# 64x64 score products, and queries and keys loaded with six tokens to a partition, in an attention and mixing kernel

## The chip, the cores and the metric

The kernel runs on one core of a Trainium2 chip. The time is that of the device in microseconds, the median of several runs of the whole kernel.

## The reference

Three stages follow each other: a windowed attention with block summaries, a token and channel mixing, and a second channel mixing. The change lies in the first.

```
# q, k, v: (2, 8, 768, 64)
k_sum = k.reshape(B, H, nb, 32, D).max(axis=3)          # nb = 24
v_sum = v.reshape(B, H, nb, 32, D).mean(axis=3)
scores_l = scale * q @ k^T, kept where |i - j| < 16, else -1e9
scores_s = scale * q @ k_sum^T + log(32)
a = softmax(concat[scores_l, scores_s])
out = a @ concat[v, v_sum]
...
h = relu(x^T @ w_tok1) @ w_tok2;  u = x + h^T
u = u + relu(u @ w_ch1) @ w_ch2
...
r = sigmoid(xr @ w_r);  out = r * (relu(xk @ w_k)^2 @ w_v)
```

## The kernel before, in words

The program writes out each engine's instructions in order and joins them by semaphores. Everything is in one core's memory; all DMAs are issued by SP, in one queue.

The attention goes over eight pairs of heads (`p`, with buffers `par` = p % 2). A pair has 12 units of 64 queries; a unit sees 96 keys of its window and 24 summary keys, 120 columns. Four units make a group `r` (three to a pair, `G` counts them through). For a pair the steps are:

- SP loads keys and queries, `load_qk` (L301), each head by itself into `kn` and `qn`: a partition gets two neighbouring tokens in each of three blocks of 256. It also loads the values, `load_v8` (L315, 96 rows of 512 floats) for the summaries and `load_vw` (L310, rows of 64 floats, windows of the values), and spreads the summed values over the units from chip memory, `spread_vs` (L321). L351 loads a piece of the weights of the mixing.
- TensorE transposes three blocks a head (`turn_k`, `turn_q`, L895) into `bK` and `bQ`. The rows of the result are token parity times the 64 features, so the copies out of PSUM take 64 rows at a time.
- DVE (L665) and ACT (L506) copy the keys to `kt`, head 0 in rows 0 to 63, head 1 in rows 64 to 127. DVE takes block maxima (`summary_keys`, L669) and cuts the windows (`cut_windows`, `add_summaries`) into `kw`. ACT copies the queries (`turn_out_q`, L498) to `qbd`, a block diagonal of both heads, whose other half stays zero from two memsets at the start (L654).
- TensorE multiplies `qbd` with `kw` (`scores`, L928), 128x128 weights for both heads of a unit, into one of two banks `bS`. DVE adds the mask and takes the negated maximum (`maxima`, L693); ACT takes exponentials (`exps`, L518). TensorE transposes them (L976) into one of two banks `bT`, ACT copies them to `aT` (L551), and TensorE multiplies by the values (L998, called AV below). DVE divides by the row sums.

On TensorE the steps of iteration `p` are, for each `r`: transposes of the exponentials of G, scores of G + 3, `turn_k` of pair p + 2 (r = 0) or `turn_q` (r = 1), the summary of the values (L918, r = 2), then AV of G. In the last two pairs products of the next stage (`hidden_tiles`, L946 to L948) fill in. SP's iteration `p` waits for the value summary of pair p to be copied, then issues L321, the loads L301 of pair p + 2 (4), L315 (2), L310 of pair p + 1 (6) and L351:

```
def pair(p, par, i=None):
    sp.wait_ge(qbank_read, 5 * p + 5)
    spread_vs(par)
    ...
        load_qk(p + 2, par)
        ...
        load_v8(p + 2)
    sp.wait_ge(av_done, 3 * p + 1)
    load_vw(p + 1, 1 - par)
```

TensorE's, SP's, ACT's and DVE's code for pairs 0 to 5 is a loop of three rounds over two pairs; the last two pairs are written out.

Of the kernel before, what the change touches and what calls it, by code (L numbers as in the profile page):

```python
# [18 lines left out]
def build_program(nc, q, k, v, w_tok1, w_tok2, w_ch1, w_ch2, mu_k, mu_r, w_k, w_v, w_r, out):  # L19
    B, NH, S, D = q.shape  # L20
    P = 128
# [31 lines left out]
    with ctx:  # L53
# [62 lines left out]
        qbd = [reg.take(f"qbd{i}", [P, NU, P]) for i in range(2)]  # L116
# [4 lines left out]
        qn = [reg.take(f"qn{i}", [P, 2, NB, P]) for i in range(2)]  # L121
        kn = [reg.take(f"kn{i}", [P, 2, NB, P]) for i in range(2)]
# [53 lines left out]
        bS, bT, bA, bQ, bK = bank[0:2], bank[2:4], bank[4:6], bank[6], bank[7]  # L176
# [120 lines left out]
        def _(sp):  # L297
            def load_qk(p, par):
                for dst, src, loaded in ((kn, k_rows, ld_k), (qn, q_rows, ld_q)):
                    for h in range(2):  # L300
                        sp.dma_start(dst[par][:, h, :, :],  # L301
                                     src[bass.ds(2 * p + h, 1)].rearrange("o p t n -> (o p) t n")
                                     ).then_inc(loaded[par], 16)
# [33 lines left out]
            def pair(p, par, i=None):  # L337
                sp.wait_ge(qbank_read, 5 * p + 5)
# [18 lines left out]
            sp.wait_ge(qbank_read, 5 * NP)  # L357
# [130 lines left out]
        def _(act):  # L488
            def turn_out_q(pp, par, h, free, banks=(bQ, bK)):


                act.wait_ge(q_turned, 2 * pp + h + 1)
                if free is not None and h == 0:
                    act.wait_ge(scores_done, free)
                for j in range(2):
                    dst = qbd[par][h * D:h * D + D, :, h * D + j:h * D + D:2]
                    src = banks[h][j * D:j * D + D, 0:NB * P].rearrange("p (u i) -> p u i", i=UQ // 2)
                    act.activation(dst, src, ACT.Copy, scale=float(D) ** -0.5).then_inc(qbank_read, 1)  # L498

            def turn_out_k(pp, free):  # L500
# [4 lines left out]
                for j in range(2):  # L505
                    act.activation(kt[D:2 * D, WIN + j:WIN + S:2], bQ[j * D:j * D + D, 0:NB * P],  # L506
                                   ACT.Copy).then_inc(kt_written, 1)
# [20 lines left out]
            act.activation(warm[:, :], qbd[0][0:D, 0, D:D + 1], ACT.Exp)  # L528
            turn_out_k(0, None)
            for h in range(2):  # L530
                turn_out_q(0, 0, h, None, bT)
# [12 lines left out]
            def pair(p, par, prep):  # L544
                for r in range(NG):
# [5 lines left out]
                    act.activation(aT[gp][:, :, :].rearrange("p u n -> p (u n)"), bT[gp][0:COLS, :],  # L551
# [72 lines left out]
            act.wait_ge(init_dve, 6)  # L624
# [27 lines left out]
        def _(dve):  # L652
            for par in range(2):
                dve.memset(qbd[par][:, :, :], 0.0).then_inc(init_dve, 1)  # L654
# [5 lines left out]
            def turn_out_k(pp, j, free):  # L660
# [4 lines left out]
                dve.tensor_copy(kt[0:D, WIN + j:WIN + S:2], bK[j * D:j * D + D, 0:NB * P]).then_inc(kt_written, 1)  # L665

            def summary_keys(pp):
                dve.wait_ge(kt_written, 4 * pp + 4)
# [14 lines left out]
            def maxima(G, r, par, free):  # L683
# [51 lines left out]
            for j in range(2):  # L735
                turn_out_k(0, j, None)
# [3 lines left out]
            maxima(0, 0, 0, None)  # L740
            maxima(1, 1, 1, None)
            for j in range(2):
                turn_out_k(1, j, 2)
# [3 lines left out]
            maxima(2, 2, 0, None)  # L747
# [9 lines left out]
            for part in range(2):  # L757
# [3 lines left out]
                for par in range(2):  # L761
                    p = 2 * i + par
                    for r in range(NG):
                        G, gp = 3 * p + r, (3 * par + r) % 2
                        if part == 0 or par == 0:
                            maxima(G + 3, r, 1 - gp, GU * G + GU)
# [6 lines left out]
                        if part == 0 and r == 0:  # L773
                            turn_out_k(p + 2, 0, 2 * p + 4)
# [370 lines left out]
```

## Time and profile before

| | |
|---|---|
| median of 3 runs | 504.31 us (503.15 to 505.6) |
| profiled execution, its span | 501.4 us |
| TensorE busy | 478.4 us (95%) |
| DVE busy | 221.7 us (44%) |
| ACT busy | 191.6 us (38%) |
| DMA | 48657 packets, 31.70 MB |

The profiled execution has no time of its own besides its span, from the first to the last instruction; the median of the runs is 2.9 us above it. The busy shares are means over stages that differ much: the attention takes the first fifth of the span. How a stage is bound is read from the windows of that stage, the queue of SP over time, and the chain of waits that ended last.

### The profile page before, as it was taken

What the parts mean: (1) busy time and instruction counts of PE and PEld (TensorE: products, weight loads), DVE (VectorE), ACT (ScalarE), POOL (GpSimd) and SP (SyncE); (2) the same over time, 40 slices, a digit from 0 to 9 for tenths busy, and PEclk for the clock granted to TensorE, in tenths of its full rate; (3) what the DMA queues carried; (4) which work ended last, traced back from release to release, by engine and by line L of the source; (5) the groups of instructions that cost most, each with busy time, mean ns of one, the idle gap of its engine ahead of it and who ended that gap; (6) DMA issues with size and microseconds to landing.
All of it is one profiled execution on the core that took longest, in us unless ns stands there. A gap on an engine that the chain in (4) does not pass through costs nothing.

```text
span 501.4 us, 8399 instructions
## 1 busy us (share of the span) xinstructions
PE 478.4 (95%) x2968; PEld 444.9 (89%) x2968; DVE 221.7 (44%) x575; ACT 191.6 (38%) x424; POOL 114.6 (23%) x98
## 2 busy tenths in 40 slices
PE   4798789998999999999999999999999999999996
PEld 4677678787999999999999999999889989989985
DVE  5598887499411141114111411456436355444521
ACT  3799887424211121112111211345455256353411
POOL 6364553285999000000000024300000000000000
PEclk9999999999999999999999999999999999999999
DMA  9999997144443100000000010000010001001001
GB/s 196 181 208 215 228 213 186 46 126 129 166 149 145 43 1 0 0 0 0 0 0 0 0 42 0 0 1 0 1 49 14 0 21 42 0 0 63 0 0 63
DMA packets 48657, 31.70 MB, mean 63 GB/s; under 512 B 21248, under 2 KB 42496, under 8 KB 48640
## 3 DMA queue, kind: packets, MB, share of 16 engines
q1 hardware_dynamic: 48640, 31.49, 26.4%
q8 instruction: 9, 0.15, 0.1%
q14 instruction: 8, 0.07, 0.1%
HBM read 27.14 MB, written 3.15 MB: 60 GB/s over the span
## 4 chain that ended last, share of the span: by engine, by line
PE 84%; SPq 5%; DMA 5%; ACT 2%; issue 2%; DVE 1%; POOL 0%; ACTq 0%; POOLq 0%
PE bank L946 26%; PE bank L947 26%; PE bank L948 26%; DMA kn<-in_k_dram 4%; SPq L301 2%; PE bank L998 1%; SPq L310 1%; DMA v<-in_v_dram 1%; PE bank L976 1%; ACT e_sb L518 1%; PE bank L1017 1%; ACT qbd L498 1%; PE bank L895 1%; SPq L321 1%; PE bank L928 1%
## 5 line engine op out<-in xcount | busy, mean ns | idle before, releaser
L845 DVE SCALAR_TENSOR_TENSOR rL<-bank,rH 128x384 fp32r<-128x384 f32 x48 | 26.7, 557 | 148.2 <-ACT rH L614 148.2
L614 ACT ACTIVATE rH<-bank 128x384 fp32r<-128x384 f32 x48 | 23.6, 492 | 163.1 <-PE bank L948 158.7
L946 PE MATMUL bank<-uH,W1H 128*128 128x384 f32 x192 | 64.8, 337 | 0.0
L947 PE MATMUL bank<-uL,W1H 128*128 128x384 f32 x192 | 64.6, 336 | 0.0
L948 PE MATMUL bank<-uH,W1L 128*128 128x384 f32 x192 | 64.4, 336 | 0.0
L947 PE MATMUL bank<-xkL,WkH 128*128 128x384 f32 x128 | 43.3, 338 | 0.0
L946 PE MATMUL bank<-xkH,WkH 128*128 128x384 f32 x128 | 43.1, 337 | 0.0
L948 PE MATMUL bank<-xkH,WkL 128*128 128x384 f32 x128 | 42.8, 335 | 0.0
L947 PEld LDWEIGHTS bank<-uL,W1H 128*128 128x128 f32 x192 | 36.1, 188 | 0.0
L948 PEld LDWEIGHTS bank<-uH,W1L 128*128 128x128 f32 x192 | 36.0, 188 | 0.0
L946 PEld LDWEIGHTS bank<-uH,W1H 128*128 128x128 f32 x192 | 36.0, 188 | 0.0
L482 POOL CAST W2aH<-stg 128x1024 fp32r<-128x1024 f32 x3 | 3.1, 1040 | 142.3 <-PE bank L948 142.3
L871 DVE SCALAR_TENSOR_TENSOR k<-bank,kr 128x384 f32<-128x384 f32 x32 | 17.8, 556 | 38.7 <-ACT kr L631 38.6
L948 PE MATMUL bank<-rH,W2aL 128*128 128x384 f32 x96 | 32.3, 336 | 0.0
L948 PE MATMUL bank<-rH,W2bL 128*128 128x384 f32 x96 | 32.3, 336 | 0.0
L946 PE MATMUL bank<-rH,W2bH 128*128 128x384 f32 x96 | 32.2, 335 | 0.0
L947 PE MATMUL bank<-rL,W2bH 128*128 128x384 f32 x96 | 32.2, 335 | 0.0
L946 PE MATMUL bank<-rH,W2aH 128*128 128x384 f32 x96 | 32.2, 335 | 0.0
L947 PE MATMUL bank<-rL,W2aH 128*128 128x384 f32 x96 | 32.2, 335 | 0.0
L631 ACT ACTIVATE kr<-bank 128x384 f32<-128x384 f32 x32 | 15.7, 489 | 43.1 <-PE bank L948 42.7
L518 ACT ACTIVATE e_sb<-s_sb,nmx 128x120 f32<-128x120 f32 x96 | 29.7, 382 | 3.3 <-DVE nmx L693 3.3
L928 PE MATMUL bank<-kw,qbd 128*128 128x120 f32 x192 | 27.6, 292 | 1.8 <-ACT qbd L498 1.6
(131 smaller groups left out, 1093.2 us busy)
## 6 DMA issues: line engine op xcount, KB each, us to landing
stg<-in_moe_w_ch_dram SPq DMA_DIRECT2D x12, 512.0 KB, 3.6
vw<-in_v_dram SPq DMA_DIRECT2D x16, 240.0 KB, 4.9
kn<-in_k_dram SPq DMA_DIRECT2D x16, 192.0 KB, 3.8
qn<-in_q_dram SPq DMA_DIRECT2D x16, 192.0 KB, 4.4
v<-in_v_dram SPq DMA_DIRECT2D x16, 192.0 KB, 5.1
out_dram<-o_sb SPq DMA_DIRECT2D x12, 256.0 KB, 2.0
stg<-in_moe_w_k_dram SPq DMA_DIRECT2D x4, 512.0 KB, 3.5
stg<-in_moe_w_v_dram SPq DMA_DIRECT2D x4, 512.0 KB, 3.4
```

The source lines that it names most:

```text
L301: sp.dma_start(dst[par][:, h, :, :], src[bass.ds(2 * p + h, 1)].rearrange("o p t n -> (o p) t n")).then_inc(loaded[par], 16)
L310: sp.dma_start(dst, src[bass.ds(2 * p + h, 1)].rearrange("o p t n -> (o p) t n")).then_inc(ld_vw[par], 16)
L321: sp.dma_start(vw[par][LOC:COLS, :, :, :].rearrange("p t h n -> p t (h n)"), vsb[par][:, :, :].rearrange("p h n -> p (h n)").unsqueeze(1) ...
L518: act.activation(e_sb[par][:, n, :], s_sb[r][:, n, :], ACT.Exp, bias=nmx[:, r, n:n + 1], scale=-1.0).then_inc(exp_done, 1)
L614: act.activation(rH[f % 2][:, :], bank[f % 2][:, 0:GR], ACT.Relu).then_inc(rh_done, 1)
L631: act.activation(kr[f % 2][:, :], bank[f % 2][:, 0:GR], ACT.Relu).then_inc(kr_done, 1)
L845: dve.scalar_tensor_tensor(out=rL[f % 2][:, :], in0=bank[f % 2][:, 0:GR], scalar=0.0, in1=rH[f % 2][:, :].bitcast(F32), op0=ALU.max, op1=A ...
L871: dve.scalar_tensor_tensor(out=k2[f % 2][:, :], in0=bank[f % 2][:, 0:GR], scalar=0.0, in1=kr[f % 2][:, :], op0=ALU.max, op1=ALU.mult).then ...
L928: ins = pe.matmul(bS[gp][:, COLS * n:COLS * n + COLS], qbd[par][:, t, :], kw[par][:, t, :], start=True, stop=True)
L946: pe.matmul(dst, wH, mH, start=start, stop=False, **more)
L947: pe.matmul(dst, wH, mL, start=False, stop=False, **more)
L948: return pe.matmul(dst, wL, mH, start=False, stop=stop, **more)
```

## The change

The diff has six parts. (1) A partition of `kn` and `qn` now holds six neighbouring tokens with both heads side by side, so a load of one head brings pieces of 64 floats. (2) A transposed block has the features of head 0 in rows 0 to 63 and of head 1 in rows 64 to 127, so one copy brings out 128 rows; the copy puts every sixth token (`in_order`). Keys: one copy by DVE and one by ACT, queries: two by ACT. (3) `qT` holds the plain queries, with no zeros, and the memsets go. (4) A score product becomes two of 64x64 weights, one a head; unit n odd has the heads' output rows swapped, which AV takes into account. (5) The scores have three banks, `bT` one; a group's scores wait for half of the maxima of the group before (`GU * (G + 2) + 2`) in place of all of those of the group before that (`GU * (G + 1) + GU`). (6) TensorE's loop over pairs is written out in full. Semaphore counts follow.

```diff
-        qbd = [reg.take(f"qbd{i}", [P, NU, P]) for i in range(2)]
+        qT = [reg.take(f"qT{i}", [P, S]) for i in range(2)]
...
-        qn = [reg.take(f"qn{i}", [P, 2, NB, P]) for i in range(2)]
-        kn = [reg.take(f"kn{i}", [P, 2, NB, P]) for i in range(2)]
+        qn = [reg.take(f"qn{i}", [P, NB, 2, 2, D]) for i in range(2)]
+        kn = [reg.take(f"kn{i}", [P, NB, 2, 2, D]) for i in range(2)]
...
-        bS, bT, bA, bQ, bK = bank[0:2], bank[2:4], bank[4:6], bank[6], bank[7]
+        bS, bT, bA, bQ, bK = bank[0:3], bank[3], bank[4:6], bank[6], bank[7]
+
+        def score_bank(r, n):
+
+            return bS[(2 * r + n % 2) % 3]
...
-        heads = "b h (t p j) d -> (b h) p t (j d)"
-        q_rows = q.rearrange(heads, t=NB, j=2)
-        k_rows = k.rearrange(heads, t=NB, j=2)
+        heads = "b h (p j) d -> (b h) p (j d)"
+        q_rows = q.rearrange(heads, j=2 * NB)
+        k_rows = k.rearrange(heads, j=2 * NB)
+
+        def turned_block(src, half, blk):
+
+            i = NB * half + blk
+            return src[:, i // 2, i % 2, :, :].rearrange("p h d -> p (h d)")
+
+        def in_order(ap, half):
+
+            return ap.rearrange("q (p i) -> q i p", i=2 * NB)[:, NB * half:NB * half + NB, :]
...
-                        sp.dma_start(dst[par][:, h, :, :],
-                                     src[bass.ds(2 * p + h, 1)].rearrange("o p t n -> (o p) t n")
+                        sp.dma_start(dst[par][:, :, :, h, :].rearrange("p t j d -> p (t j) d"),
+                                     src[bass.ds(2 * p + h, 1)].rearrange("o p (i d) -> (o p) i d", d=D)
...
-                for j in range(2):
-                    dst = qbd[par][h * D:h * D + D, :, h * D + j:h * D + D:2]
-                    src = banks[h][j * D:j * D + D, 0:NB * P].rearrange("p (u i) -> p u i", i=UQ // 2)
-                    act.activation(dst, src, ACT.Copy, scale=float(D) ** -0.5).then_inc(qbank_read, 1)
+                dst = in_order(qT[par][:, :], half)
+                act.activation(dst, columns(banks[half], dst), ACT.Copy, scale=float(D) ** -0.5).then_inc(qbank_read, 1)
...
-            for par in range(2):
-                dve.memset(qbd[par][:, :, :], 0.0).then_inc(init_dve, 1)
...
-                for n in range(GU):
-
-
-                    dve.tensor_tensor_reduce(out=s_sb[r][:, n, :], in0=bS[par][:, COLS * n:COLS * n + COLS],
+                for n in (0, 2, 1, 3):
+                    c = COLS * (n // 2)
+                    dve.tensor_tensor_reduce(out=s_sb[r][:, n, :], in0=score_bank(r, n)[:, c:c + COLS],
...
-                    t = GU * r + n
-                    ins = pe.matmul(bS[gp][:, COLS * n:COLS * n + COLS], qbd[par][:, t, :], kw[par][:, t, :],
-                                    start=True, stop=True)
+                    t, c = GU * r + n, COLS * (n // 2)
+                    for h in range(2):
+                        rows, to = slice(h * D, h * D + D), slice((h + n) % 2 * UQ, (h + n) % 2 * UQ + UQ)
+                        ins = pe.matmul(score_bank(r, n)[to, c:c + COLS], qT[par][rows, t * UQ:t * UQ + UQ],
+                                        kw[par][rows, t, :], start=True, stop=True)
...
-                        scores(p + 1, 1 - par, r, 1 - gp, GU * (G + 1) + GU)
+                        scores(p + 1, 1 - par, r, GU * (G + 2) + 2)
...
-            with pe.Fori(0, NP // 2 - 1) as i:
-                for par in range(2):
-                    pair(2 * i + par, par, True)
-            for par in range(2):
-                pair(NP - 2 + par, par, False)
+            for p in range(NP):
+                pair(p, p % 2, p < NP - 2)
```

What SP issues at the head of its loop over the pairs (`vw_72` and `kn_77` are the buffers of even pairs; ISA and REGISTER_ALU rows are waits and register work). Before:

```order
L321 DMA vw_72<-vsb_83 24x12x130
L341 ISA
L301 ISA
L301 DMA kn_77<-in_k_dram 128x3x128
L301 ISA
L301 DMA kn_77<-in_k_dram 128x3x128
L301 DMA qn_75<-in_q_dram 128x3x128 x2
L344 REGISTER_ALU
L315 DMA v_79<-in_v_dram 96x512 x2
```

and now:

```order
L334 DMA vw_72<-vsb_83 24x12x130
L354 ISA
L314 ISA
L314 DMA kn_77<-in_k_dram 128x6x64
L314 ISA
L314 DMA kn_77<-in_k_dram 128x6x64
L314 DMA qn_75<-in_q_dram 128x6x64 x2
L357 REGISTER_ALU
L328 DMA v_79<-in_v_dram 96x512 x2
```

The order is the same; each load of keys or queries has six pieces of 64 floats a partition in place of three of 128.

On ACT, from the copy of the keys to the copy of the third group's transposed exponentials, in the loop over the pairs. Before:

```order
L506 ACTIVATE kt<-bank 64x384 x2
L551 ACTIVATE aT_88<-bank 120x512
L515 ISA
L518 ACTIVATE e_sb_86<-s_sb_89,nmx 128x120 x4
L492 REGISTER_ALU
L498 ACTIVATE qbd_68<-bank 64x12x32 x4
L551 ACTIVATE aT_87<-bank 120x512
```

and now:

```order
L521 ACTIVATE kt<-bank 128x3x128
L565 ACTIVATE aT_88<-bank 120x512
L529 ISA
L532 ACTIVATE e_sb_86<-s_sb_89,nmx 128x120 x4
L509 REGISTER_ALU
L513 ACTIVATE qT_68<-bank 128x3x128 x2
L565 ACTIVATE aT_87<-bank 120x512
```

Two copies of keys are one, four of queries are two, each with 128 rows; nothing else moves.

On TensorE, the first iteration over a pair, from the first group's transposes. Before, in the loop:

```order
L976 MATMUL bank<-ident,e_sb_85 120x128 x4
L922 ISA
L923 ISA
L925 ISA
L928 MATMUL bank<-kw_71,qbd_69 128x120 x4
L901 ISA
L903 ISA
L895 MATMUL bank<-ident,kn_77 128x128 x6
L991 ISA
L992 ISA
L998 MATMUL bank<-vw_72,aT_87 64x65 x8
L976 MATMUL bank<-ident,e_sb_86 120x128 x4
```

and now, written out:

```order
L988 MATMUL bank<-ident,e_sb_85 120x128 x4
L940 MATMUL bank<-kw_71,qT_69 64x120 x8
L905 MATMUL bank<-ident,kn_77 128x128 x6
L1011 MATMUL bank<-vw_72,aT_87 64x65 x8
L988 MATMUL bank<-ident,e_sb_86 120x128 x4
L940 MATMUL bank<-kw_71,qT_69 64x120 x8
```

Four score products of a group are eight, with 64 rows of output each, in the same places, and the waits and register rows of the loop are gone or carried by the products.

## Rows read from the trace of the kernel before

**Rows 1.** The page: span, slices of TensorE and of DMA, DMA packets.

```profile
span 501.4 us, 8399 instructions
...
PE   4798789998999999999999999999999999999996
...
DMA  9999997144443100000000010000010001001001
...
DMA packets 48657, 31.70 MB, mean 63 GB/s; under 512 B 21248, under 2 KB 42496, under 8 KB 48640
```

**Rows 2.** The timeline of SP, its queue: start us, us, line, transfer, count.

```profile
16.57 1.02 SPq L301 DMA_DIRECT2D kn<-in_k_dram  x2
...
26.21 1.31 SPq L301 DMA_DIRECT2D kn<-in_k_dram  x2
...
56.99 1.13 SPq L301 DMA_DIRECT2D kn<-in_k_dram  x2
...
60.49 3.59 SPq L310 DMA_DIRECT2D vw<-in_v_dram  x6
...
65.97 1.16 SPq L301 DMA_DIRECT2D kn<-in_k_dram  x2
```

**Rows 3.** The views of L301, L310, L321: ns of one issue, min/median/max.

```profile
L301 SPq DMA_DIRECT2D kn<-in_k_dram x16: 387/438/645, 0.8 to 66.6; - x16
...
L310 SPq DMA_DIRECT2D vw<-in_v_dram x48: 317/374/2298, 6.0 to 81.3; - x48
...
L321 SPq DMA_DIRECT2D vw<-vsb x8: 822/840/997, 15.2 to 81.9; - x8
```

**Rows 4.** Waits of SP from 0 to 100 us: in total, times, longest.

```profile
SPq L321 <- ACT qbd L498: 3.3, 4, 0.9
```

**Rows 5.** Waits of TensorE from 20 to 80 us: in total, times, longest.

```profile
PE bank L895 <- DMA kn<-in_k_dram: 4.1, 5, 1.6
```

**Rows 6.** One round, by windows: busy of PE, PEld, DVE, ACT, POOL; clock; DMA.

```profile
46.00:57.00 11.00, 9.24 (x106) 7.94 (x106) 9.04 (x42) 9.40 (x26) 5.79 (x6) 1.00 1.23 211
```

**Rows 7.** The chain that ended last, 60 to 98 us: start, us, what.

```profile
66.62 4.77 DMA kn<-in_k_dram
...
75.41 0.43 ACT qbd L498
...
76.95 0.52 ACT qbd L498
...
79.46 0.89 PE bank L928 x8
```

**Rows 8.** The same chain in the first 32 us.

```profile
5.55 5.95 DMA v<-in_v_dram
```

**Rows 9.** Windows by what is in flight; the last figure is GB/s.

```profile
2.00:6.00 4.00, 1.51 (x6) 1.14 (x6) 2.62 (x7) 1.11 (x3) 3.25 (x12) 1.00 0.88 254
...
10.00:12.00 2.00, 2.00 (x11) 2.00 (x11) 0.33 (x3) 0.00 (x0) 0.43 (x1) 1.00 1.39 177
...
39.00:41.00 2.00, 1.68 (x19) 1.43 (x15) 1.37 (x7) 1.94 (x8) 0.81 (x1) 1.00 1.16 274
...
53.00:55.00 2.00, 1.94 (x22) 1.69 (x18) 1.60 (x5) 1.88 (x6) 0.57 (x1) 1.00 1.34 198
...
81.00:83.00 2.00, 2.00 (x26) 1.52 (x25) 1.80 (x12) 0.62 (x3) 1.33 (x2) 1.00 0.99 206
...
86.00:88.00 2.00, 2.00 (x26) 1.56 (x24) 1.03 (x9) 2.00 (x7) 0.00 (x0) 1.00 0.99 337
```

**Rows 10.** Groups of instructions, 0 to 170 us: count, busy us, mean ns.

```profile
L498 ACT ACTIVATE qbd<-bank 64x384 f32<-64x384 f32 x32 | 16.6, 519 | 1.7 <-PE bank L895 1.2
...
L665 DVE COPY kt<-bank 64x384 f32<-64x384 f32 x16 | 8.9, 555 | 4.3 <-PE bank L895 3.0 <-issue 0.9
...
L588 ACT ACTIVATE u<-bank 128x384 f32<-128x384 f32 x16 | 7.9, 492 | 14.3 <-PE bank L1017 14.3
...
L693 DVE CUSTOM_DVE_ANT_0 s_sb<-bank,mask 128x120 f32<-128x120 f32 x96 | 21.2, 276 | 6.8 <-ACT e_sb L518 3.1 <-PE bank L928 2.8 <-issue 0.8
```

More of the change, by code:

```diff
@@ L488, in _, with columns, turn_out_q @@
         def _(act):
-            def turn_out_q(pp, par, h, free, banks=(bQ, bK)):
-                act.wait_ge(q_turned, 2 * pp + h + 1)
-                if free is not None and h == 0:
+            def columns(bank, dst):
+                src = bank[:, 0:NB * P]
+                return src if len(dst.shape) == 2 else src.rearrange("q (i p) -> q i p", i=NB)
+            def turn_out_q(pp, par, half, free, banks=(bQ, bK)):
+                act.wait_ge(q_turned, 2 * pp + half + 1)
+                if free is not None and half == 0:
                     act.wait_ge(scores_done, free)
-                for j in range(2):
-                    dst = qbd[par][h * D:h * D + D, :, h * D + j:h * D + D:2]
-                    src = banks[h][j * D:j * D + D, 0:NB * P].rearrange("p (u i) -> p u i", i=UQ // 2)
-                    act.activation(dst, src, ACT.Copy, scale=float(D) ** -0.5).then_inc(qbank_read, 1)
+                dst = in_order(qT[par][:, :], half)
+                act.activation(dst, columns(banks[half], dst), ACT.Copy, scale=float(D) ** -0.5).then_inc(qbank_read, 1)
             def turn_out_k(pp, free):
@@ L504, in turn_out_k @@
                     act.wait_ge(kw_ready, free)
-                for j in range(2):
-                    act.activation(kt[D:2 * D, WIN + j:WIN + S:2], bQ[j * D:j * D + D, 0:NB * P],
-                                   ACT.Copy).then_inc(kt_written, 1)
+                dst = in_order(kt[:, WIN:WIN + S], 1)
+                act.activation(dst, columns(bQ, dst), ACT.Copy).then_inc(kt_written, 1)
             def turn_out_vs(p, par):
@@ L526, in _ @@
             act.wait_ge(init_dve, 1)
-            act.activation(warm[:, :], qbd[0][0:D, 0, D:D + 1], ACT.Exp)
+            act.activation(warm[:, :], kt[0:D, 0:1], ACT.Exp)
             turn_out_k(0, None)
             for h in range(2):
-                turn_out_q(0, 0, h, None, bT)
+                turn_out_q(0, 0, h, None, bA)
             exps(0, 0, 0)
@@ L681, in add_summaries, with maxima @@
                                 ks[:, :].unsqueeze(1).to_broadcast([P, NU, NSUM])).then_inc(kw_ready, 1)
-            def maxima(G, r, par, free):
+            def maxima(G, r, free):
                 dve.wait_ge(init_pool, 4)
@@ L733, in high_wt @@
                 dve.tensor_copy(hi, halves(stg[par][:, 0:512])).then_inc(wh_done, 1)
-            for j in range(2):
-                turn_out_k(0, j, None)
+            turn_out_k(0, None)
             summary_keys(0)
@@ L739, in _ @@
             add_summaries(0, 0)
[L740 to L743, printed above, removed]
+            maxima(0, 0, None)
+            maxima(1, 1, None)
+            turn_out_k(1, 2)
             summary_keys(1)
@@ L746, in _ @@
             add_summaries(1, 1)
-            maxima(2, 2, 0, None)
+            maxima(2, 2, None)
             dve.wait_ge(ld_mu, 32)
@@ L765, in _ @@
                         if part == 0 or par == 0:
-                            maxima(G + 3, r, 1 - gp, GU * G + GU)
+                            maxima(G + 3, r, GU * G + GU)
                         if part == 1 and 3 * par + r == 2 * NG - 1:
@@ L779, in _ @@
                         invert(G, r)
-                        if part == 0 and r == 0:
-                            turn_out_k(p + 2, 1, 2 * p + 4)
-                        elif part == 0 and r == 1:
+                        if part == 0 and r == 1:
                             cut_windows(par, 3 * p + 3)
@@ L892, in _, with turn @@
         def _(pe):
-            def turn(src, dst):
+            def turn(src, half, dst):
                 for blk in range(NB):
-                    ins = pe.transpose(dst[:, blk * P:blk * P + P], src[:, blk, :], ident[:, :])
+                    ins = pe.transpose(dst[:, blk * P:blk * P + P], turned_block(src, half, blk), ident[:, :])
                 return ins
```

56 lines of the change are left out of this document (30 added, 26 removed).

## Prediction

> **What bounds the kernel now.** I began with the page [rows 1]. TensorE stands at 9 in nearly every slice of the span, but not in the first eight, and there the DMA row stands at 9 six times and once at 7; after that it falls. The change touches only the attention, which lies in the first eight slices (100 us), so the question is what ends last there.
>
> Next the queue of SP over time [rows 2]. From 16.6 us on it issues without a pause: a round for one pair of heads is four loads of queries and keys (L301), two of L315, six of L310, one of L351, one of L321, and then the next L301. Of five rounds the first begins with L301 at 26.21 and the last at 65.97 us: 39.76 us for four rounds, 9.94 us each. In the shortest, from 56.99, the six L310 take 3.59 us, though a typical one needs 0.374 us [rows 3], 2.2 us for six: SP is held back inside L310, even there. The list of SP's waits [rows 4] has 3.3 us on ACT in four waits and little else, while TensorE in the same stretch waits for `kn` to land [rows 5]. In one round (46 to 57 us) the 16 DMA engines show a share of 1.23 (over 1, since packets overlap) at 211 GB/s, and DVE and ACT are busy 9.0 and 9.4 us of 11 [rows 6]. So the DMA engines set the pace of the attention, ACT stands close behind, and TensorE's products cost nothing there. This holds until the keys of the last pair land at 71.4 us; the chain then runs over ACT and TensorE [rows 7]. The chain of the first 32 us says the same of the start: it is the eight loads L301 and one of L315, then 5.95 us until `v8` lands behind them [rows 8], then POOL, TensorE, ACT and L321.
>
> **The change, part by part.**
>
> *Loads.* Each `kn`/`qn` load still moves 128 x 384 x 4 = 196.6 kB, but as 128x6x64 in place of 128x3x128: 768 pieces of 256 B in place of 384 of 512 B. Over 32 loads that is 12,288 more packets. The trace has both sizes. Where L301's loads are in flight the rate is 254 GB/s at the start and 274 at 39 to 41 us; where it is L310, whose rows are 64 floats (256 B), the rate is 177 GB/s in the first of four windows and 198 in the last, mean of the four 185.5 [rows 9]. A load takes 0.77 and 0.72 us by the first pair, 0.75 on average, and 1.06 by the second: **+0.31 us a load**. The upper end is 1.11 less 0.72, 0.39; the lower is from 81 to 83 us, where 256 B rows arrive with no queue behind them at 206 GB/s: 0.95 less 0.75, 0.20. I take 0.31, since the loads run in a full queue as those windows do.
>
> The Trainium skill ("DMA: Bandwidth & Descriptors", Why small descriptors are slow) counts 11 cycles for a 256-byte descriptor, 3 of them fixed; by the same count 512 bytes take 19, so two small ones cost 22 against 19. That would be an estimate of +0.12 us a load and, with the other terms below, 506.8 us. The rows differ from it by more, 185.5 against some 264 GB/s, and I go by the rows; the page's Specifications ("≥512 B" for line rate) do agree with them.
>
> How many loads count: eight stand ahead of `v8` in the first chain (8 x 0.31 = 2.5 us), and 22 from the restart at 16.57 us to the keys of the last pair (five pairs of four, then two): 6.8 us. Together **+9.3 us**.
>
> *Issue.* The other cost of a load is SP's time. L301 takes 0.438 us; L321, a form whose two sides don't split alike, takes 0.840 [rows 3]. The new loads may stay at the first or go to the second, as their source is now one row of 768 pieces; then +0.40 us each. The shortest round, from 56.99 to 65.97, has 9.0 us, of which 3.59 - 2.24 = 1.35 is the hold in L310 [rows 2, 3]; the other 7.6 and 1.6 more make 9.2 us, under the 9.94 + 4 x 0.31 = 11.2 us that the DMA engines need. So I cost it at nothing, hidden by the drain; at the start 8 x 0.40 = 3.2 would take the place of 2.5.
>
> *Copies out of PSUM.* ACT's four copies of queries become two, its two of keys one; DVE's two become one. Now one of queries takes 519 ns and one of DVE's 555 [rows 10]; ACT's copies of keys have the form of the first. The new ones have 128 rows by 384 and write at a step of six elements. Below: 492 ns, the contiguous 128x384 copy of L588 [rows 10]; above I allow twice 519, since no row has this step. At 519 a round saves 3 x 0.52 on ACT, 0.56 on DVE, all under cover of the loads, which is why I count none of it for the rounds. In the last round the chain holds all four L498, from 75.41 to 77.47 us [rows 7]: two fall away, **-1.0 us**. The keys' copy there isn't in the chain. At twice the price the term is 0.
>
> *Score products.* Per group of four units, four products 128x120 (two instructions each) become eight of 64x64 tiles. Now 8 instructions take 0.89 us in the chain, 111 ns each [rows 7]. If two tiles run at a time it stays so; all four at once, 0.45; one after another, 1.78. Only three groups are in the chain, all after the last keys, the first at 79.46 us: 3 x 0.44 = -1.3 to 3 x 0.89 = +2.7 us. I take 0, between the ends.
>
> *The rest at nothing.* The two memsets of `qbd` ran while the first keys were loading. Scores now wait for half of the maxima of the group before, where they waited for all of the group two back; behind that wait on TensorE stand the products of AV, for which DVE's row sums wait. They have had the time of AV and four transposes since; TensorE is idle for `kn` there besides [rows 5]. Uncovered it is two of a group's four maxima, 2 x 0.276 us [rows 10]. `bT` has one bank, but its last reader is awaited anyway. TensorE's loop is written out; nothing in the rows makes a branch or its code a wait of the chain.
>
> Sum: 9.3 - 1.0 = +8.3 us on a span of 501.4, 509.7. The median of the runs, 504.31, is 2.9 above the span, and I carry that over: **512.6 us**.
>
> **The rivals.**
>
> *A light price.* The loads cost 0.20 each, as at 81 to 83 us: 6.0 - 1.0, 509.3 us. For it: their source is contiguous, as that of L310 isn't. Against: that window has no full queue.
>
> *TensorE serialises the small products.* +0.89 us in three groups, +2.7: 515.3 us. At the start the sum of `v` is awaited anyway. For it: both heads write one bank. The Trainium skill ("TensorEngine Tiling (Array Packing)", Gotcha 1 and Key Properties) says that different row tiles cannot access one PSUM bank simultaneously, and that a change of mode drains the engine. No row here has two row tiles, so no run shows it yet.
>
> *Issue and drain add up*, 0.31 + 0.40 a load over 30 loads, 21.3 - 1.0: 524.6 us. Against it: SP was held back in each round.
>
> *The loads are as fast as before*: the engines' time goes by bytes. Then only the copies show: 503.3 us. Against it: 185 against 264 GB/s.
>
> *The other side, faster.* A partition's six tokens are 1,536 B in one piece in DRAM. If the read side sets the price, a load goes towards the 337 GB/s of the 1 KB rows at 86 to 88 us [rows 9], 0.58 us: -0.17 x 30 = -5.1, -1.0, 498.2 us. It decides once a load is 0.05 us cheaper than now (-1.5 - 1.0 = -2.5 us). Against it: the writes are 256 B pieces, and L310's rate is low with the same.
>
> **Chances.** The forecast (price near 0.31) 0.48, light price 0.20, serial products 0.12, issue added 0.04, no change of the loads 0.09, faster loads 0.07. A measurement of this kernel tells about 0.5% (2.5 us) from no change. Slower: 0.48 + 0.20 + 0.12 + 0.04 = 0.84; same 0.09; faster 0.07. The range leaves out the last three cases, 0.20. Its low end is 504.3 + 6.0 - 1.0 - 1.3 = 508.0, and half a microsecond less for DVE's copy, which lets the last queries turn earlier: 507.5. Its high end is 504.3 + 12.0 (0.40 a load, the issue's price) - 1.0 + 2.7 = 518.0, and 1.0 for copies at twice their price, and I go to 521 for a part of the added issue.
>
> **What would show it.** The page: packets up by 12,288 to some 60,945, those under 512 B from 21,248 to some 45,800. The queue: rounds of SP at 11.2 us in place of 9.94, the last keys landing near 80.7. The windows with only L314 in flight near 185 GB/s. ACT: two copies of about 0.52 us where there were four. TensorE: longer waits for `kn`, 16 score instructions in about 0.9 us. The chain after the last keys' landing some 1 us shorter. I am wrong if the rounds stay at 10 us, or if the rounds are no longer set by loads but by ACT (the strided copies) or the queue's issue.

## The result and the profile after

The change makes the kernel slower: 509.32 us (median of four runs, 508.25 to 510.68) against 504.23 for the kernel before, run beside it; the ratio is 1.0105, 95% interval 1.008 to 1.0131. The direction and the range held; the likeliest time was 3.3 us too high, and the median fell on the rival with the light price for the loads (509.3).

The page of the kernel after, its span, slices, clock and packets:

```profile
span 506.8 us, 8693 instructions
...
PE   4778868999999999999999999999999999999996
DMA  9999998415444200000000001000010001001001
DMA packets 60948, 31.76 MB, mean 63 GB/s; under 512 B 45824, under 2 KB 54784, under 8 KB 60928
```

The packets are up by 12,291 and those under 512 B by 24,576, as the sizes say [rows 1]. The DMA row stands at 9 to the sixth slice as before, then at 8 and 4 where it stood at 7 and 1. Past the attention the time is the same (403.4 and 403.3 us, below).

The timeline of SP's queue after (start, us, line, transfer, count); these answer to [rows 2]:

```profile
17.27 1.38 SPq L314 DMA_DIRECT2D kn<-in_k_dram  x2
...
27.97 1.36 SPq L314 DMA_DIRECT2D kn<-in_k_dram  x2
...
61.71 1.36 SPq L314 DMA_DIRECT2D kn<-in_k_dram  x2
...
65.86 4.36 SPq L323 DMA_DIRECT2D vw<-in_v_dram  x6
...
72.19 1.37 SPq L314 DMA_DIRECT2D kn<-in_k_dram  x2
```

The restart is the first load behind the start (17.27 us, 16.57 before): it is 0.7 later. From there to the last pair's load it is 54.92 us, 49.40 before: +5.5 over five rounds. SP is still held inside the six loads of `vw` (L323 here, L310 before). What one issue of the new form takes (ns, min/median/max):

```profile
L314 SPq DMA_DIRECT2D kn<-in_k_dram x16: 549/590/907, 0.8 to 73.0; - x16
```

0.59 us: neither the old 0.44 nor the 0.84 of the row that I set beside it [rows 3].

The chain that ended last, from the last load of keys to the first product of the next stage, `u`'s transposes (L1027); it answers to [rows 7]:

```profile
73.02 3.77 DMA kn<-in_k_dram
...
76.84 0.87 PE bank L905 x6
...
81.27 0.95 DVE ks L684
...
83.07 0.42 DVE u L730
...
83.52 0.40 PE bank L928 x2
...
84.58 0.58 PE bank L988 x4
85.16 0.57 PE bank L940 x16
85.73 0.43 PE bank L958
...
103.42 0.48 PE bank L1027 x3
```

And the same two ends in the chain before (`kn` turned; `u` turned), which are not among the rows above:

```profile
71.52 0.87 PE bank L895 x6
...
98.13 0.48 PE bank L1017 x3
```

The last keys are turned at 76.84 in place of 71.52, +5.32 us, and that is the whole of the difference: from there to `u`'s transposes it is 26.58 us after and 26.61 before, and from there to the end 403.4 and 403.3. The +5.32 are 0.70 of the start, +5.52 of the rounds, and -0.90 from the issue of the last load of keys to its landing. So the last round gave nothing back, though two copies fell away in it. That is two changes that cancel: to the transposes of the exponentials (L988) it is 7.74 us from the keys (84.58), 7.36 before (78.88), and from there to `u`'s transposes 18.84 us in place of 19.25. The copies themselves (groups of lines to 170 us, with mean ns of one):

```profile
L513 ACT ACTIVATE qT<-bank 128x384 f32<-128x384 f32 x16 | 12.6, 891 | 1.3 <-PE bank L905 1.1
...
L521 ACT ACTIVATE kt<-bank 128x384 f32<-128x384 f32 x8 | 7.0, 871 | 11.4 <-PE bank L905 11.4
L680 DVE COPY kt<-bank 128x384 f32<-128x384 f32 x8 | 6.8, 846 | 8.6 <-PE bank L905 8.4
```

One copy with 128 rows takes 0.85 to 0.89 us where one with 64 took 0.52 to 0.56 [rows 10]. Two of 0.89 still beat four of 0.52, but by 0.3 us and not by half.

TensorE's waits from 20 to 80 us (in total, times, longest) show what is late next:

```profile
PE bank L905 <- DMA kn<-in_k_dram: 7.5, 5, 2.0
PE bank L928 <- DVE u L730: 3.9, 3, 1.4
```

The wait for keys has gone from 4.1 to 7.5 us [rows 5], and the wait ahead of L928, the product that sums v, is 4.4 us with the 0.5 that is put down to POOL, where it was 2.5 before (L918 there), in three times, none over 0.9. The row names DVE's `u`; but in the kernel's code L928 waits for two things only, POOL's sum of v and ACT's copies of the queries. In the last round the copies end at 82.21, and the sum ends only at 83.46, just ahead of L928's 83.52:

```profile
82.78 0.68 POOL L454 TENSOR_TENSOR v<-v 96x128 f32<-96x128 f32 x1 [0.25 <-POOL v L451]
```

One more row, of the windows from 27 to 67 us (busy of PE, PEld, DVE, ACT, POOL; clock; DMA share; GB/s), before and after:

```profile
27.00:67.00 40.00, 34.99 (x401) 29.83 (x401) 34.42 (x162) 36.51 (x99) 22.59 (x21) 1.00 1.19 216
```

```profile
27.00:67.00 40.00, 30.91 (x441) 23.06 (x434) 29.67 (x143) 29.64 (x78) 21.01 (x20) 0.87 0.99 198
```

Every engine is less busy in the same 40 us, the DMA engines too (share 1.19 to 0.99), and the granted clock of TensorE is 0.87 in place of 1.00.

What one round is made of shows in the chain. Before, in three of the four rounds from 26.21 us on it goes from the landing of the keys over TensorE and ACT back to SP, since SP's spread of the summed values (L321) waits for ACT's copies of the queries; only in the last it stays in SP's queue. One such round:

```profile
37.26 3.86 DMA kn<-in_k_dram
41.25 0.87 PE bank L895 x6
...
43.90 1.24 ACT e_sb L518 x4
45.14 0.45 ACT qbd L498
```

After, two of the four rounds from 27.97 go this way and two stay in SP's queue:

```profile
62.52 3.12 DMA kn<-in_k_dram
...
65.69 0.88 PE bank L905 x6
...
68.35 1.24 ACT e_sb L532 x4
69.59 1.55 ACT qT L513 x2
```

### The profile page after: what moved, and what is told of

Its sections match the earlier page's. It is cut to its first block, busy times and chain, and to the rows that moved or that the text cites. A ratio compares the mean times of both kernels' runs of the same rounds, so it can differ in the third digit from the quotient of the medians.

```text
span 506.8 us, 8693 instructions
## 1 busy us (share of the span) xinstructions
PE 475.0 (94%) x3160; PEld 434.7 (86%) x3160; DVE 217.3 (43%) x565; ACT 186.6 (37%) x400; POOL 115.2 (23%) x98
## 4 chain that ended last, share of the span: by engine, by line
PE 84%; SPq 6%; DMA 4%; ACT 2%; issue 2%; DVE 1%; POOL 1%; ACTq 0%; DVEq 0%; POOLq 0%
PE bank L958 26%; PE bank L959 26%; PE bank L960 26%; SPq L314 3%; DMA kn<-in_k_dram 2%; SPq L323 2%; PE bank L1011 2%; DMA v<-in_v_dram 1%; PE bank L988 1%; PE bank L1027 1%; ACT e_sb L532 1%; ACT qT L513 1%; PE bank L905 1%; SPq L328 1%; SPq L334 1%
## 5 line engine op out<-in xcount | busy, mean ns | idle before, releaser
L958 PE MATMUL bank<-W2aH,k2H 128*128 128x512 f32 x72 | 28.3, 393 | 0.0
```

Of the source, the lines that this page charges most:

```text
L958: pe.matmul(dst, wH, mH, start=start, stop=False, **more)
```

## Experiments

A profile is one execution. Of kernels with before's loads and no load added, the profiles show five rounds of 49.40 us (before), 50.75 (u1), 51.22 (c1) and 52.96 (s1), and a restart at 15.72 (c1) to 16.57 us, so a difference of less than 1 to 2 us between two profiles tells little.

Two theories stood after the result. **Pieces:** the loads drain more slowly because they have 768 pieces of 256 B in place of 384 of 512 B. **Issue:** SP needs 0.15 us more for each load, 30 loads. Beside them stood the question what each other part was worth.

Two matrix products with the identity, one a head, stand for each transpose in the first four runs (24 instructions in 1.53 us in place of 6 in 0.87), since these layouts hold a block's two heads apart; the first of them is the control.

**Control, m0.** The kernel after, with only this:

```
-                    ins = pe.transpose(dst[:, blk * P:blk * P + P], turned_block(src, half, blk), ident[:, :])
+                    for h in range(2):
+                        ins = pe.matmul(dst[h * D:h * D + D, blk * P:blk * P + P], turned_block(src, half, blk, h),
+                                        ident[:, :], start=True, stop=True)
```

> Control for the three runs beside it: the changed kernel with its loads in 256 B pieces, but each block is transposed by two products with the identity, one a head, so that the heads need not lie side by side in kn and qn. TensorE has more to do (48 instructions a turn pair for 12), in a stage where it waits for keys. Both theories: rounds of SP stay at 11.05 us as in the changed kernel, the whole within +0 to +3 us of it (509 to 512 us), the excess in the last round, where nothing covers TensorE.

509.27 us (ratio 1.0092, 1.0065 to 1.012), that of the kernel after, so what follows can be read against it.

**512 B pieces, m1.** The same source, as contiguous as before, written in three pieces of 512 B a partition (the index of the blocks to be turned follows):

```
-                        sp.dma_start(dst[par][:, :, :, h, :].rearrange("p t j d -> p (t j) d"),
-                                     src[bass.ds(2 * p + h, 1)].rearrange("o p (i d) -> (o p) i d", d=D)
+                        sp.dma_start(dst[par][:, :, h, :, :].rearrange("p t j d -> p t (j d)"),
+                                     src[bass.ds(2 * p + h, 1)].rearrange("o p (t n) -> (o p) t n", t=NB)
```

> As the control, but a head's load comes in three pieces of 512 B a partition (six neighbouring tokens, still read from one contiguous stretch). Theory P (the number and size of pieces set the round): 12,288 fewer packets, rounds back to about 10.0 us, 5 us less than the control. Theory Q (SP's time to issue the new form of load, 0.59 us in place of 0.44, sets it): the form keeps its contiguous source, so the issue stays near 0.59 us, the rounds near 10.9 us, within 1 us of the control.

505.37 us (1.0028, 1.0009 to 1.0048): 3.9 us of the 5.2 between m0 and the kernel before, and SP's time for an issue had hardly changed. Issue, min/median/max, first in m0 and then in m1:

```profile
L314 SPq DMA_DIRECT2D kn<-in_k_dram x16: 550/592/751, 0.8 to 73.0; - x16
```

```profile
L314 SPq DMA_DIRECT2D kn<-in_k_dram x16: 550/611/1294, 0.8 to 70.6; - x16
```

That separates the two: the size of the pieces costs by itself. (m1's profiled execution took 507.7 us, 2.3 above the median, so its trace may understate what the larger pieces give.) The price is seen best where only these loads are in flight, from 3 to 6 us, in m0 and in m1 (last figure GB/s):

```profile
3.00:6.00 3.00, 0.72 (x8) 0.76 (x10) 0.00 (x0) 0.10 (x1) 2.51 (x7) 1.00 1.07 232
```

```profile
3.00:6.00 3.00, 1.29 (x12) 1.32 (x14) 0.00 (x0) 0.11 (x1) 2.52 (x7) 1.00 0.94 268
```

196.6 kB at 232 and at 268 GB/s are 0.85 and 0.73 us: +0.11 us a load, 3.4 over 30 loads, near the 3.9 measured. By the Trainium skill ("DMA: Bandwidth & Descriptors", Why small descriptors are slow) it was to be 0.12, the estimate that I had set aside for the rate of L310's rows.

**One piece, m2.** Both heads apart, a partition's six tokens in one piece of 1,536 B (the index of the blocks follows here too):

```
-        kn = [reg.take(f"kn{i}", [P, NB, 2, 2, D]) for i in range(2)]
+        kn = [reg.take(f"kn{i}", [P, 2, 2 * NB, D]) for i in range(2)]
-                        sp.dma_start(dst[par][:, :, :, h, :].rearrange("p t j d -> p (t j) d"),
-                                     src[bass.ds(2 * p + h, 1)].rearrange("o p (i d) -> (o p) i d", d=D)
+                        sp.dma_start(dst[par][:, h, :, :].rearrange("p i d -> p (i d)"),
+                                     src[bass.ds(2 * p + h, 1)].rearrange("o p n -> (o p) n")
```

> As the control, but a head's load is one piece of 1,536 B a partition, 128 packets a load, contiguous on both sides. Theory P: less drain than any, rounds at or below 9.9 us, 5 to 7 us less than the control. Theory Q: the issue falls to about 0.41 us as for L328 (a load of the same two-dimensional form), rounds near 10.2 us, about 4 us less than the control. Tells P from Q only together with the run in 512 B pieces.

503.44 us (0.9988, 0.9958 to 1.0019): 1.9 us under m1, with 40,471 packets and 0.383 us an issue. The changed products and banks with the best loads come out level with the kernel before, not ahead of it. Two causes moved together here, so this run doesn't part them.

**Before's loads and token order, m3.** The loads bring the pieces of the kernel before; the copies keep 128 rows but write at a step of two elements:

```
-        heads = "b h (p j) d -> (b h) p (j d)"
+        heads = "b h (t p j) d -> (b h) p t (j d)"
...
-            return ap.rearrange("q (p i) -> q i p", i=2 * NB)[:, NB * half:NB * half + NB, :]
+            return ap.rearrange("q (i j) -> q j i", j=2)[:, half, :]
```

> As the control, but with the loads of the kernel before (two tokens in each of three blocks, 512 B pieces, contiguous in kn), so the 128-row copies write at a step of two elements, not six. Both theories: rounds near 9.95 us, 4 to 5 us less than the control. On the copies: if the step of six costs, ACT's 128x384 copy falls from 0.89 us to about 0.5; if it is the number of rows, it stays at 0.89.

504.83 us (1.001, 0.9989 to 1.0031), level with the kernel before. The copies (groups to 170 us):

```profile
L512 ACT ACTIVATE qT<-bank 128x384 f32<-128x384 f32 x16 | 7.9, 520 | 3.3 <-PE bank L905 3.0
```

So 128 rows cost what 64 did, and 0.37 us of the 0.89 come from the step of six elements. m3 has m1's size of piece and 0.435 us an issue in place of 0.61; 0.5 us between them is inside the spread of both, though issue, order in DRAM and copies all differ. From 3 to 6 us the rate is 265 GB/s with m3's pieces of 512 B, which lie apart in DRAM, and 268 with m1's, which lie side by side: at this size the order in DRAM shows no difference.

**Issue alone, i1.** The kernel before, with two tiny loads in front of each round's loads of keys:

```
+                    sp.wait_ge(ld_tiny, 32 * p + 32)
+                    for n in range(2):
+                        sp.dma_start(tiny[:, n, :], wr_rows[0:16, 0, 0:16]).then_inc(ld_tiny, 16)
                     load_qk(p + 2, par)
```

> The kernel before with two tiny loads more in each round of SP, ahead of L301 (16 pieces of 64 B each into an unused tile), and two at the start: SP's time alone, some 0.8 us a round, with 32 packets. Theory P (the DMA engines' drain sets the round, SP's issue is hidden): rounds stay at 9.94 to 10.1 us, the whole within 1 us of the kernel before. Theory Q (SP's time counts in full): rounds 10.7 us, the whole +4.5 to +5.5 us, 509 us.

506.45 us (1.0071, 1.0049 to 1.0092), and neither theory as stated. The timeline of its queue shows that the two took 1.1 us here, not the 0.8 of the expectation, and with the gap behind them 1.2 to 1.5 us in each of five rounds:

```profile
47.57 1.11 SPq L349 DMA_DIRECT2D tiny<-in_moe_w_r_dram  x2
48.93 1.01 SPq L303 DMA_DIRECT2D kn<-in_k_dram  x2
```

The restart is 1.3 us later (17.91): of the 0.9 us added ahead of the first loads 0.3 is left when SP issues its first spread (15.49 in place of 15.18), and the 1.1 just ahead of the restart shows in full. Five rounds take 51.19 us, 1.8 more than before's, of 5.5 or more added: a third at most. By the profile alone that third isn't shown, as c1's rounds are as long with nothing added; the times show that the whole costs 2.5 us or more, so "at nothing" was too low. The tiny loads also had to be waited for, which the kernel after doesn't do.

**The loop written out, u1**, the kernel before with only the last edit of the diff:

```
-            with pe.Fori(0, NP // 2 - 1) as i:
-                for par in range(2):
-                    pair(2 * i + par, par, True)
-            for par in range(2):
-                pair(NP - 2 + par, par, False)
+            for p in range(NP):
+                pair(p, p % 2, p < NP - 2)
```

> The kernel before with TensorE's loop over pairs written out, nothing else. If the code of TensorE is fetched behind its work: no difference (504 us). If fetching code among the loads holds it up: +1 us or more, with 16 KB fetches in the attention going from 2 to some 6.

504.44 us (1.002, 1.0001 to 1.0039): between nothing and 0.4% slower.

**Small products alone, s1.** u1, with the score products cut to 64x64 tiles from the diagonal of `qbd`, both heads into the same bank, each head always to the same rows:

```
-                    ins = pe.matmul(bS[gp][:, COLS * n:COLS * n + COLS], qbd[par][:, t, :], kw[par][:, t, :],
-                                    start=True, stop=True)
+                    for h in range(2):
+                        rows = slice(h * D, h * D + D)
+                        ins = pe.matmul(bS[gp][rows, COLS * n:COLS * n + COLS], qbd[par][rows, t, rows],
+                                        kw[par][rows, t, :], start=True, stop=True)
```

> The kernel before, TensorE's loop written out, and each score product made as two of 64x64 weights from the diagonal of qbd, both heads into the same bank and without the swap of rows for odd units: two of four tiles in use. If two tiles run side by side 16 instructions take about 0.9 us in the chain; if the swap and the third bank make no difference, 0.57 us as in the changed kernel; one after another, 1.7 us. The whole: -1 to +3 us against the run that is only written out.

505.70 us (1.0032, 1.0008 to 1.0056), 1.3 over u1. Its profiled execution took 506.98 us, with five rounds of 52.96 us; what made them long stays open. The chain, where the group's products and the next stage's first stand:

```profile
82.35 0.97 PE bank L930 x16
83.32 0.43 PE bank L948
```

Eight products with two instructions each in 0.97 us: 61 ns each where the larger ones took 111 [rows 7]; at 111 one after another would be 1.78 us. That fits two tiles at a time, though both write one bank. And the first 128x128 product behind them takes 0.43 us where it took 0.24.

**Products, banks and waits with before's loads and copies, c1.** u1, with `qT` in place of `qbd`, the eight products with a unit's two heads changing places from unit to unit (`(h + n) % 2`), `score_bank`, one `bT`, and after's waits, but the copies with 64 rows:

```
-                    dst = qbd[par][h * D:h * D + D, :, h * D + j:h * D + D:2]
-                    src = banks[h][j * D:j * D + D, 0:NB * P].rearrange("p (u i) -> p u i", i=UQ // 2)
+                    dst = qT[par][h * D:h * D + D, j:S:2]
+                    src = banks[h][j * D:j * D + D, 0:NB * P]
```

> The changed kernel with its loads and copies undone: loads of 512 B pieces and copies of 64 rows as before, into plain queries; 64x64 products, banks, waits and the written-out loop as in the change. Both theories: rounds 9.94 us, the last keys at 71.5 us; the products save 0.1 us in each of three groups of the chain: 503.5 to 504.5 us. If the new waits or banks cost anything, it shows as more than 504.5 us.

504.20 us (1.0023, 0.9998 to 1.0048); u1, its base, has 504.44. Its chain:

```profile
79.43 0.57 PE bank L931 x16
80.00 0.43 PE bank L949
```

16 instructions take 0.57 us, as in the kernel after: with the heads changing places four tiles are used, and it is 0.4 us quicker than s1. Neighbouring units also go to different banks here and not in s1, and no run parts the two. Of 0.32 us gained on 0.89 a group the next product takes 0.19 back. Everything in the change but the loads and the copies is worth nothing that these runs tell (the interval allows up to 0.5% slower).

**The order of the copies, h1.** The kernel after; each copy walks a partition's three tokens first, so it writes three floats side by side and reads PSUM at a step of 128:

```
-            return ap.rearrange("q (p i) -> q i p", i=2 * NB)[:, NB * half:NB * half + NB, :]
+            return ap.rearrange("q (p i) -> q p i", i=2 * NB)[:, :, NB * half:NB * half + NB]
```

> The kernel after, but each copy out of PSUM walks its 128x3 elements the other way round: three tokens of a partition first, written side by side, then on by six; the reads now go through PSUM at a step of 128 elements, the writes no longer jump 24 bytes each. Theory (what makes a copy 0.85 to 0.89 us in place of 0.52 is the jump of every write): copies of 0.5 to 0.6 us, and since two of them stand in the chain behind the last keys, 509.3 - 2 x 0.35 = 508.6 us; the rounds stay at 11.0 us, as they are set by the loads. Rival (any step beyond two elements costs, on the read side too): copies of 0.85 us or more and 509.3 us. Rival (the copies set the rounds as well, in part): the rounds of SP shorter too and 507 us or less.

508.53 us (1.0111, 1.0088 to 1.0134). The copies fell as the theory had it:

```profile
L513 ACT ACTIVATE qT<-bank 128x384 f32<-128x384 f32 x16 | 8.4, 566 | 2.8 <-PE bank L905 2.3
...
L521 ACT ACTIVATE kt<-bank 128x384 f32<-128x384 f32 x8 | 4.6, 570 | 11.9 <-PE bank L905 11.9
L680 DVE COPY kt<-bank 128x384 f32<-128x384 f32 x8 | 4.5, 561 | 8.8 <-PE bank L905 8.5
```

The time did not: by ratios (1.0111 against 1.0105) nothing came of it, and from the keys (76.91) to the first L1027 (103.59) it is 26.68 us, as long as with the slow copies (26.58). The rounds take 54.76 us, as before the edit, though SP's waits for ACT's copies of the queries fell from 2.4 to 0.8 us: the slow copies did not set the rounds. So it is the jump of 24 bytes at each write that costs a copy 0.3 us, a read of PSUM at a step of 512 bytes costs almost none of it, and something else holds the last round. The Trainium skill ("SBUF — State Buffer", Specifications (TRN2), the row on cachelines: "need ≥2 hits per line for full bandwidth", lines of 16 bytes) fits what the runs show: full speed at a step of 8 bytes, not at one of 24.

**The sum of v behind AV, v1.** h1, with one call moved:

```
-                    if prep and r == NG - 1:
-                        sum_vs(p + 2, 3 * (p + 2) + 1)
...
                     ins.then_inc(av_done, 1)
+                    if prep and r == NG - 1:
+                        sum_vs(p + 2, 3 * (p + 2) + 1)
```

> The run with the copy order changed (508.53 us), and on TensorE the product that sums v (L928 there) stands behind the group's products of AV in place of ahead of them. In the kernel after and in that run it waits until 83.5 to 83.8 us for the sums of POOL, which start when v8 lands, behind the last four loads of queries and keys; AV, the row sums and the transposes of the next group stand behind it. Theory (this wait has eaten what the two copies less gave back in the last round): from the landing of the last keys to the first L1027 25.2 to 25.8 us in place of 26.6 to 26.7, the rounds as they were, and 507.4 to 507.9 us. Rival (DVE's work on the keys, ks and kw, which stands ahead of the normalising u there, ends no earlier, and AV waits for it): from the keys to L1027 26.4 us or more and 508.5 us. Rival (the sums come too late for the copies of ACT and the spread that starts SP's next round): rounds of over 11.1 us and 509.5 us or more.

The profiled execution (507.44 us) did what the theory said: keys at 76.48, first L1027 at 102.22, 25.74 us, 0.9 less than in h1, in a span of 505.6. The rival that AV waits for DVE's `u` fell: AV began at 81.92 and that `u` at 82.56. The chain now runs over `v`:

```profile
79.94 1.27 POOL v L449
...
82.26 0.69 POOL v L454
...
83.00 0.40 PE bank L928 x2
```

The median, 508.36 us (1.0098, 1.007 to 1.0126), is only 0.2 under h1's, above the 507.4 to 507.9 that I gave it; a gain of 0.9 can't be told from none by these runs. Even now the transposes behind L928 wait for POOL, which starts when `v8` lands behind the last four loads.

**One piece with the other copies, h2 and g1.** h2 is m2 with h1's copies. g1 is c1 with one piece of 1,536 B:

```
-        heads = "b h (t p j) d -> (b h) p t (j d)"
+        heads = "b h (p t j) d -> (b h) p t (j d)"
-                    dst = qT[par][h * D:h * D + D, j:S:2]
-                    src = banks[h][j * D:j * D + D, 0:NB * P]
+                    dst = qT[par][h * D:h * D + D, j:S:2].rearrange("q (p t) -> q p t", t=NB)
+                    src = banks[h][j * D:j * D + D, 0:NB * P].rearrange("q (t p) -> q p t", t=NB)
```

> The run with one piece of 1536 B a partition and head (503.44 us), with the copies out of PSUM walking the three tokens of a partition first, as in the run before. Theory (there ACT and DVE stand close behind the loads, with copies of 0.87 us): the copies fall to some 0.55 us, the tail gains 0.7 and the rounds up to 1 us over the five: 501.7 to 502.7 us. Rival (reads at a step of 128 elements cost as much): 503.4 us. Rival (the rounds are set by the DMA queue alone): 502.7 us, the rounds at 10.45 us as they were.

> The run with before's loads and 64-row copies but the changed products, banks and waits (504.2 us), with one piece of 1536 B a partition and head in the loads: the tokens of a partition are six in a row, and a copy reads PSUM at a step of 128 elements so that it still writes at a step of two. Theory (number and size of the pieces set the rounds): the rounds fall from 10.24 to under 10.0 us, packets from some 48,660 to some 40,470, and the time to some 502.5 us. Rival (with pieces of 512 B the queue is held back by ACT and L323's rows already): 504.2 us and rounds of 10.2 us. Rival (reads at that step cost the copies 0.35 us each, and with six copies of a round on ACT they set the rounds): 505 us or more.

503.45 us (1.0009, 0.9985 to 1.0034) and 503.13 us (1.0001, 0.9982 to 1.002). In h2 the faster copies bring nothing, like in h1, and the theory of 501.7 to 502.7 fell. In g1 the rounds are 51.19 us, c1's are 51.22: with 0.37 us an issue and 8,192 packets fewer they are no shorter, where the theory wanted under 10.0 us each. Its waits of SP from 0 to 100 us:

```profile
SPq L314 <- PE bank L1004: 3.4, 2, 2.7
SPq L325 <- ACT qT L502: 2.9, 5, 0.8
```

SP waits for ACT and TensorE as well, as it does in c1 (3.9 and 3.7 us), and in both the chain of the first rounds runs over ACT's exponentials and copies. With before's copies, pieces larger than 512 B gain nothing that shows. No version that was run beats the kernel before.

## Why the prediction was right, and where it was off

- **Right: smaller pieces make the kernel slower, through the loads.** m0 to m1 shows it with nothing else changed: 3.9 us of 5.2.
- **Off: the price of a load.** The step that failed is "+0.31 us a load", taken from the windows where L310's rows are in flight. Measured alone, 256 B pieces cost +0.11 us. The lower bound, 0.20, which carried the light rival, was nearer but came from L310's rows too. Why these are slower stays open: they lie apart in DRAM and stand beside other small transfers, but no run varied either with pieces of 256 B, and with 512 B the order in DRAM showed no difference (m1, m3). That the median met 509.3 is in part chance: it had 6.0 for the loads and -1.0 for the copies; the profile has +6.2 at SP (start and rounds), -0.9 from the last issue to its landing, and 0 from there on.
- **Off: "the DMA engines set the pace", and "TensorE's products cost nothing there".** The chain of a round ran before as after over TensorE and ACT too, in three rounds of four and in two of four; SP's 3.3 us of waits on ACT [rows 4] were its sign. The share of the DMA engines, 1.23, was no sign of a limit: from 27 to 67 us it is 0.98 in m0 and in m1 alike, 1.19 before and 0.99 after. The round came out at 11.06 us against 11.2, but less than half of its growth is the pieces' price; the last keys were there at 76.8 us, not near 80.7.
- **Off: the start.** Of 2.5 us, 0.7 came (1.5 against u1 and c1, whose restarts are at 15.75 and 15.72). Eight loads at 224 GB/s from 3 to 6 us in place of 253 are 0.10 us each, 0.8 together. SP's issues are slower at the same time (`v8`'s first load is issued at 6.85 in place of 5.02), so the start doesn't part the two. The chain stays on SP's issues until 7.94 us and then waits less for `v` than the 5.95 of before [rows 8]:

```profile
6.85 1.05 SPq L328
7.94 4.27 DMA v<-in_v_dram
```

- **Off: issue at nothing.** I said that the drain hides it. i1's time shows that SP's added time counts, by its profile with a third at most in the rounds. In the kernel after they grew by 1.10 us each. Pieces make 0.48 of that: five rounds take 54.86 us in m0 and 52.44 in m1, and 4 x 0.11 = 0.44 agrees. For issue I estimate 0.2 from i1 (4 x 0.15, a third), and m1 to m3 (51.41) gives 0.2 too, though the copies differ there. The other 0.4 stays open; u1's five rounds take 50.75 us where before's took 49.40, so single profiles differ by that much, and against c1 the growth is 0.74 a round, which the two nearly fill.
- **Copies, -1.0.** Inside its range but for the wrong reason. At 0.89 us in place of 0.52, the saving in the last round was 0.3 (4 x 0.52 against 2 x 0.89), plus what shorter handovers gave: `aT`'s copy behind them began 5.2 us after the keys in place of 6.0. Then the sum of v ate it and 0.4 us more (7.74 against 7.36 to L988), a wait that the prediction did not name. It names POOL's sums only at the start. v1 supports this in its profile, not in its median.
- **Products at 0.** -0.32 us a group and +0.19 for the product behind them: -0.4 over three groups, as the 18.84 against 19.25 us show. The rival that TensorE serialises them fell: both heads write one bank, in s1 with 61 ns an instruction. The Trainium skill's sentence ("TensorEngine Tiling (Array Packing)", Gotcha 1) that different row tiles cannot access one bank simultaneously, isn't borne out where they write different partitions of it; what its Key Properties say of a drain at a change of mode agrees with the 0.43 us.
- **The rest at nothing.** Held: c1 and u1 are level.

## What to carry to other kernels

A price for a transfer is safest read from the same transfer, with only the size of its pieces changed: 256 B pieces cost 0.11 us a load more than 512 B pieces, and the rows of another transfer with pieces of 256 B had suggested 0.31. A copy with all 128 rows costs no more than one with 64, but look at the step of its writes in bytes before counting the gain. A high share of the DMA engines doesn't prove that they set a round: look at what the chain passes through inside it. And follow every load of a queue to its reader: by the profiles, what was saved behind the keys was waited for again behind v.

## What the runs showed of the hardware that I had not expected

- The jump of each write: ACT and DVE copies of 128x384 from PSUM take 0.52 and 0.56 us at a step of two floats (m3), 0.87 to 0.89 and 0.85 at a step of six (after), and 0.57 and 0.56 where three floats lie side by side and the read is at a step of 128 (h1).
- One and the same load of 196.6 kB takes SP 0.38 us to issue as one piece a partition (m2), 0.44 as three from rows that lie apart (before), and 0.59 to 0.61 as six or three pieces from a contiguous source (after, m1). The number of pieces is not what sets it.
- 16 instructions of 64x64 score products take 0.57 us where the heads change places and the bank changes from unit to unit, and 0.97 us where neither does. The 128x128 product behind either takes 0.43 us, 0.24 behind the large ones.
- In the kernel after, TensorE waits longer for keys, and its granted clock (the column before the DMA share) falls after two of these waits to the lower of its two levels, 1.2 GHz (0.50). From 32 to 33 us TensorE was busy 0.22 us, from 43 to 44 us 0.02 us; the clock stood at 0.50 from 34 to 36 us and from 44 to 50 us:

```profile
34.00:37.00 3.00, 3.00 (x37) 2.33 (x36) 1.43 (x4) 1.79 (x4) 1.04 (x2) 0.55 1.26 200
46.00:49.00 3.00, 3.00 (x34) 2.24 (x31) 1.43 (x4) 1.79 (x5) 1.27 (x2) 0.50 0.92 152
```

Four transposes of the exponentials take 1.05 us at 34.98, 0.58 to 0.60 at the full clock. With before's loads and copies (c1) the clock is 1.00 from 27 to 67 us. That the low clock made the rounds longer isn't shown: m0's are as long (54.86 us) with a clock of 0.96 in place of 0.87.
